# Second round's last counts and chain steps one slot earlier, second expert's token pieces turned at the first expert's last product

## What is computed

```python
def _moe_ref(x, w_gate, w1, w2):            # N, D = 1536, 512; E, F = 8, 1024
    cap = N // E                            # 192 tokens for each expert
    logits = x @ w_gate
    order = np.argsort(-logits.flatten())
    ...                                     # best (token, expert) pair first; full experts are passed over
    for e in range(E):
        mask = assigned == e
        h = np.maximum(x[mask] @ w1[e], 0.0)
        out[mask] = h @ w2[e]

def _moe2_ref(x, w_in, w_out, alpha):       # d_ff = 2048
    h = x @ w_in
    g = np.maximum(h, 0.0) + alpha * np.minimum(h, 0.0)
    return g @ w_out
```

## Time and profile before

| | us |
|---|---|
| median of 3 runs | 648.62 (648.44 to 649.32) |
| the profiled execution | 646.13 |
| its span, first to last instruction | 644.4 |

### The profile page before, as it was taken

How to read it: one execution, slowest core, us unless ns; L and a number is a source line. 1 busy time by engine, 2 the same in 40 slices (tenths; PEclk the granted TensorE clock), 3 DMA queues, 4 the chain that set the end, 5 groups by cost and what they waited for, 6 DMA issues and landing times.

```text
span 644.4 us, 12853 instructions
## 1 busy us (share of the span) xinstructions
PE 620.3 (96%) x4926; PEld 554.2 (86%) x4933; DVE 418.6 (65%) x1148; ACT 299.7 (47%) x704; POOL 195.7 (30%) x212
## 2 busy tenths in 40 slices
PE   7899999989999999999999999999999999999994
PEld 4788897558899888899999888999988989999994
DVE  8688887988576979844759798438577520045551
ACT  5877784111122655532246554322566542346652
POOL 5988870010110342121113431201234420123322
PEclk9999999999999999999999999999999999999998
DMA  7477765525350143027103510470017610000001
GB/s 257 148 262 267 257 197 165 180 91 198 110 226 2 66 149 122 2 79 264 45 2 106 188 43 1 138 246 2 2 66 260 239 44 14 1 0 2 1 1 49
DMA packets 31284, 72.36 MB, mean 112 GB/s; under 512 B 2940, under 2 KB 3000, under 8 KB 31224
## 3 DMA queue, kind: packets, MB, share of 16 engines
q1 hardware_dynamic: 27232, 60.69, 27.3%
q0 software_dynamic: 2048, 6.29, 3.3%
q10 hardware_dynamic: 1944, 4.56, 2.0%
HBM read 65.22 MB, written 6.32 MB: 111 GB/s over the span
## 4 chain that ended last, share of the span: by engine, by line
PE 81%; DVE 5%; ACT 1%; issue 0%; POOL 0%; POOLq 0%; ACTq 0%; DVEq 0%
PE bank L1511 21%; PE bank L1500 20%; PE bank L1418 13%; PE bank L1409 13%; PE bank L1334 3%; DVE beats L906 3%; PE bank L1253 2%; PE bank L1217 1%; PE bank L1199 1%; PE bank L1387 1%; PE bank L1365 1%; PE bank L1274 1%; DVE ties L915 1%; PE bank L1349 0%; POOL out L603 0%
## 5 line engine op out<-in xcount | busy, mean ns | idle before, releaser
L580 POOL TENSOR_TENSOR wi_lo<-w_in,wi_hi 128x512 fp32r<-128x512 f32 x64 | 85.7, 1342 | 278.8 <-ACT wi_hi L706 278.8
L906 DVE TENSOR_SCALAR beats<-rank_row,key 128x512 bf16<-128x512 f32 (+11 forms) x173 | 105.7, 636 | 13.0 <-PE bank L1336 13.0
L1511 PE MATMUL bank<-wo_hi,g_lo 128*128 128x512 f32 x192 | 76.0, 396 | 0.0
L1511 PE MATMUL bank<-wo_lo,g_hi 128*128 128x512 f32 x192 | 75.8, 395 | 0.0
L1511 PE MATMUL bank<-wo_hi,g_hi 128*128 128x512 f32 x192 | 75.5, 393 | 0.0
L1156 DVE SCALAR_TENSOR_TENSOR g<-bank,g_neg 128x384 f32<-128x384 f32 x64 | 35.5, 555 | 57.4 <-ACT g_neg L760 57.1
L758 ACT ACTIVATE g_neg<-bank 128x384 f32<-128x384 f32 x64 | 31.4, 491 | 79.8 <-PE bank L1500 79.8
L1500 PE MATMUL bank<-y_hi,wi_hi 128*128 128x384 f32 x256 | 58.2, 349 | 1.3 <-DVE g L1156 1.3
L642 ACT ACTIVATE prob<-neg_s,neg_max 128x260 f32<-128x260 f32 x96 | 48.9, 510 | 18.7 <-DVE neg_max L817 17.3
L732 ACT ACTIVATE h_t<-bank 128x192 f32<-128x192 f32 x64 | 21.1, 330 | 74.1 <-PE bank L1409 74.1
L1500 PE MATMUL bank<-y_hi,wi_lo 128*128 128x384 f32 x256 | 55.3, 337 | 0.0
(11 more groups left out here) (163 smaller groups left out, 1340.7 us busy)
## 6 DMA issues: line engine op xcount, KB each, us to landing
w_a<-moe_w SPq DMA_DIRECT2D x8, 1024.0 KB, 5.1
w_a<-moe_w SPq DMA_DIRECT2D x4, 2048.0 KB, 10.2
w_b<-moe_w SPq DMA_DIRECT2D x8, 1024.0 KB, 5.1
w_b<-moe_w SPq DMA_DIRECT2D x4, 2048.0 KB, 10.3
k_raw<-k_t SPq DMA_DIRECT2D x11, 512.0 KB, 5.1
q_raw<-q_t SPq DMA_DIRECT2D x11, 512.0 KB, 3.7
w_in<-moe_w_in SPq DMA_DIRECT2D x8, 512.0 KB, 5.3
w_out<-moe_w_out SPq DMA_DIRECT2D x8, 512.0 KB, 5.6
```

Source lines behind the costliest of these rows:

```text
L580: nc.gpsimd.tensor_tensor(out=wi_lo[:, f % 2, :, :], in0=w_in[:, :, f * P:(f + 1) * P], in1=wi_hi[:, f % 2, :, :].bitcast(F32), op=ALU.sub ...
L906: return nc.vector.tensor_scalar(out=beats[:, c % 3, lo:hi], in0=rank_row[:, lo:hi], scalar1=key[:, c:c + 1], scalar2=None, op0=op)
L1511: last = nc.tensor.matmul(DOWN_BANK[t][:, :], a[:, f % 3, t * P:(t + 1) * P], w[:, f % 2, :], start=(f == 0 and n == 0), stop=(f == FC - 1 ...
```

## The change

On PE, in expert 0: the counts of blocks 8 to 11 move to the places behind products 4 (8 and 9) and 5 (10 and 11) instead of products 4, 5 (9 and 10) and 6 (11); in the numbers of the code, done = 5 and 6 instead of 5, 6 and 7. `across(1)` moves from done = 8 to 7, `before_and_loads(1)` from 8.5 to 8, `pick_tokens(1)` from 10 to 9.5. The turning of expert 1's tokens is cut in two: piece 0 goes into the middle of product 11 (done = 11.5), piece 1 stands right behind it, and the four matmuls on zeros are gone. On ACT the copy of piece 0 stands behind `store_keys(2)`, before the last `y_hi` copy, and that of piece 1 behind `load_row(2)`. On DVE the second part of `picks(1)` no longer has `y_rest(0, 0)` in front of it.

```diff
@@ scalar engine
-            def copy_x(r):
+            def copy_x(r, pieces=range(TURNS)):
...
-                for k, (t, rows) in enumerate(ROWS[e]):
+                for k in pieces:
+                    t, rows = ROWS[e][k]
                     act.wait_ge(x_turned, TURNS * r + k + 1)
...
-                if r < 2:
+                if r == 0:
                     copy_x(r)
...
                     if r == 0 and m == 2:
                         store_keys(2)
+                        copy_x(1, (0,))
                 if r == 0:
                     load_row(2)
+                    copy_x(1, (1,))
@@ vector engine, experts(0)
                     fill_expert(1)
-                    picks(1, PARTS[0])
+                    for tiles in PARTS:
+                        picks(1, tiles)
                     y_rest(0, 0)
-                    picks(1, PARTS[1])
                     token_numbers(1)
@@ tensor engine
+            def turn_piece(r, k):
+
+                j, e = r // 2, r % 2
+                t, rows = ROWS[e][k]
+                pe.wait_ge(gathered[e][k], 16 * (j + 1))
...
+                for c in range(DC):
+                    last = nc.tensor.transpose(x_bank(r, k)[:, c * width:(c + 1) * width], x_g[rows, t, c * P:(c + 1) * P],
+                                               ident[rows, rows])
+                last.then_inc(x_turned, 1)
+
             def turn_tokens(r):
...
+                for k in range(TURNS):
+                    turn_piece(r, k)
...
-            SECOND_ROUND = {1: (3,), 2: (4,), 3: (5, 6), 4: (7,), 5: (8,), 6: (9, 10), 7: (11,)}
+            SECOND_ROUND = {1: (3,), 2: (4,), 3: (5, 6), 4: (7,), 5: (8, 9), 6: (10, 11)}
...
+                    if done == 7:
+                        across(1)
                     if done == 8:
-                        across(1)
-                    if done == 8.5:
                         before_and_loads(1)
-                    if done == 10:
+                    if done == 9.5:
                         pick_tokens(1)
                     if done == 11:
                         turn_keys(2)
+                    if done == 11.5:
+                        turn_piece(1, 0)
...
                 if j == 0:
-                    keep_clock(4, DOWN_BANK[2])
-                    turn_tokens(1)
+                    turn_piece(1, 1)
```

More of the change, by code:

```diff
@@ L1370, in _ @@
             pe.wait_ge(consts_ready, CONSTS)
-            def turn_tokens(r):
[L1374 to L1389, removed]
+            def turn_piece(r, k):
+                j, e = r // 2, r % 2
+                t, rows = ROWS[e][k]
+                pe.wait_ge(gathered[e][k], 16 * (j + 1))
+                if r == 0:
+                    pe.wait_ge(row_copied, 3 + k + 1)
+                elif e:
+                    wait_above(pe, o_copied, GT * j)
+                else:
+                    pe.wait_ge(y_copied, DC * r - 1 + k)
+                    if k == 0 and j < NG - 1:
+                        pe.wait_ge(keys_copied, KEYS_BESIDE_FFN[j - 1] - 1)
+                width = rows.stop - rows.start
+                for c in range(DC):
+                    last = nc.tensor.transpose(x_bank(r, k)[:, c * width:(c + 1) * width], x_g[rows, t, c * P:(c + 1) * P],
+                                               ident[rows, rows])
+                last.then_inc(x_turned, 1)
+            def turn_tokens(r):
+                for k in range(TURNS):
+                    turn_piece(r, k)
             def product(r, k):
```

## The result

The changed kernel takes 649.22 us (median of 20 runs, 647.05 to 651.91) against 647.74 us for the kernel before, measured beside it (20 runs, 646.15 to 649.32). The ratio is 1.0026 with a 95% interval of 1.0015 to 1.0036: slower by 1.7 us (1.0 to 2.3), where 0.75 us less was forecast.

The account below looks back on a forecast made before the run. PE, busy 96% of the span, was taken to bound the kernel. The filler's 0.81 us less 0.05 for the tie gave 0.75, so 648.62 becomes 647.9 us; range 646.9 to 649.1, the forecast's own 647.6 to 648.1.

Parts of the forecast that it names:

- the quarter of a microsecond forecast at count 11 and at `across`: Moved routing steps in expert 0: inputs ready 0.25 us ahead at both places, so PE does not wait.
- they take nothing off PE: Routing steps one slot earlier in expert 0: same sum on PE up to product 11, only slack of 1.30 us.
- the gathers in time: Middle of product 11: piece 0 landed 1.4 us before PE asks, 0.0 with the slowest landing.
- the filler's 0.8 us: Seam from expert 0 to 1: gain 0.8 us, exactly the matmuls on zeros; expert 1 starts at 176.5 against 177.28.
- What is late next: Third round's first count: keys' load issued 0.4 us later, a tie with PE at 182.3, costing 0 to 0.1 us.
- It shares them after the change too: Keys' load beside expert 1's weights: DMA engines shared as before, earlier weights leave the keys' share alone.
- the 6.2 us: Keys' load for the third round: issue to landing taken over unchanged from the kernel before.
- the gain is eaten at count 0: Rival, third round's first count: keys' load alone 0.8 us late, 648.6 us, no change; chance 13%.
- a load issued later than 175.3: Sign of being wrong: `load_row` going out after 175.3, where the keys' load was forecast near 175.2.
- Keys stored late and holding ACT: Rival, ACT before expert 1: late store delays `load_row(2)` and piece 1's copy; 649.8 us or more; chance 8%.
- The clock at the seam: Rival, start of expert 1: without zeros products 0 to 3 run at 1.2 GHz, 5.4 us more, 653.3; chance 2%.
- More than the filler gained: Rival, gathers at the seam: landing later without the profiler, so gain 1.2 to 1.7 us, 646.9; chance 17%.

Follow-up runs that it names:

- turning only: The changed kernel with the second round's routing steps put back to their old places; ratio 1.0030 to the kernel before.
- zeros gone: The kernel before with only the four matmuls on zeros behind product 11 of expert 0 taken out; ratio 0.9991.
- keys first: The changed kernel with w2 of expert 1 issued behind the keys' load and `load_row(2)` ahead of the last `y_hi` copy; ratio 0.9975 to the kernel before.
- both pieces: keys first with piece 1 also turned in the middle of product 11, its copy ahead of the last `y_hi` copy; 645.7 us, ratio 0.9965 to the kernel before.
- minimal: The kernel before with zeros gone, `load_row(2)` ahead of the last `y_hi` copy and w2 behind that copy, without moved steps, pieces or cut copies; ratio 0.9993.
- the first four experiments: The kernel before without zeros, or with only the steps moved; the changed kernel with steps put back, or with w2 held back; ratios 0.9991, 1.0015, 1.0030, 1.0006.
- w2 behind keys: The changed kernel with one wait on SP, so w2 of expert 1 is issued behind the last `y_hi` copy; 647.89 us, ratio 1.0006 to the kernel before.
- before with w2 behind: The kernel before with only w2 of expert 1 issued behind the last `y_hi` copy of expert 0; ratio 1.0001.
- before again: The kernel before, unchanged, run once more for a second trace; no ratio given, first count 10.49 us behind the issue of the keys' store.

## Why the prediction was wrong

**What held.** That PE bounds the stretch; that all of the moved steps find their inputs (the quarter of a microsecond forecast at count 11 and at `across` sufficed); that they take nothing off PE; the gathers in time; the seam cheaper by the filler's 0.8 us (0.89 in the trace); no fall of the clock at the seam; that the keys' load is what comes late next, with no room left.

**The step that failed** is in "What is late next": "It shares them after the change too", and with it the 6.2 us taken over for a load that was issued in another order. The load took 7.5 and 7.7 us and PE waited 1.9 and 2.1 us where I had 0 to 0.1. The first trace's 1.89 us are 1.26 for the later landing (7.46 against 6.2), 0.44 for a term that I had mis-sized (from DVE's start on the landed keys to the count are 1.34 us, 183.94 to 185.28, where I put 0.9, although I took 1.4 us a block a few sentences later), and some 0.2 for a load issued 0.5 to 0.6 us later instead of 0.4 and the tie. Even with the old 6.2 us the count would have been at 10.4 behind the store and the gain about 0.1. The sum was 0.8 gained at the seam and 1.9 lost at the count, 1.1 us slower (11.63 against 10.49 behind the keys' store; 11.84 in the second trace), which lies in the interval of the runs, 1.0 to 2.3. I had seen that both transfers share the engines, and that the weights move up by 1.3 us. I had not looked at which of them was issued first: before, the keys went out 0.2 us ahead of w2; after, 1.7 behind. I named this cost as a rival ("the gain is eaten at count 0") and priced it as a load 0.8 late. DVE started 1.5 us later than forecast (10.29 us behind the store, where 2.6 and 6.2 make 8.8), and the longer first block came on top. One of my own signs of being wrong, a load issued later than 175.3, was met by a hair (175.32), but that was the small part.

The Trainium skill's page "DMA: Bandwidth & Descriptors", section "Queues, rings and completion order", on which I leaned, says that each engine takes turns between queues packet by packet. The rows disagree with how I read it: 1.20 MB of weights moved in 3 us, 104% of the engines' time, with the keys' load already issued. Once both move they agree with it: in the kernel before, 178 to 180 us, 100 packets of the keys passed beside 99 of the weights. The keys' share is three times as large since their packets hold 6 KB against 2 KB (0.61 MB against 0.20). The same section says that SP and ACT have no descriptor generator of their own. A common one that works in order of issue would explain that w2 ahead of the keys delays them. It would not by itself explain that their first bytes come 3.8 us behind their issue with w2 0.4 us ahead (turning only), 1.7 ahead (the change) and 0.1 behind (zeros gone). No run here tests it. That w2's place costs the time is shown; how it does so stays open.

**The other rivals.** Keys stored late and holding ACT: not seen; the load went out at once behind product 11 in both traces. The clock at the seam: in thirteen traces no window of 5 us between 155 and 235 us is below 1.00, with seams that hold 0.7 us of idle time and waits of up to 2.1 us. More than the filler gained: not in the changed kernel, whose two traces show 0.8 us at the seam and no more.

**What stays open.** The runs move more than the traces in some kernels: 1.6 us against 0.8 for keys first, 2.3 against 1.4 for both pieces, 1.7 against 1.1 for the change; in minimal they move less, 0.5 against 0.9. The granted clock of single runs lies between 0.986 and 0.998, and in the traces the low stretches, apart from the kernel's end, are at 15 to 30 or 145 to 155 us, ahead of all that is edited. The mean over the runs was 0.9918 for the changed kernel and 0.9940, 0.9927 and 0.9932 for the kernel before on three chips. Within one kernel a run whose mean clock is lower by 0.001 is some 0.3 us longer. An estimate with that slope, all runs taken to one clock, leaves the change 0.9 us slower (0.4 to 1.3, against the 33 runs of before that came with the first experiments), keys first 1.3 faster, minimal 0.8 faster and both pieces 1.9 faster. So about half of the 1.7 us may go with the clock and not with the wait. On the chip of the first four experiments the kernels with pieces turned in product 11 had the lower clock (0.9921 and 0.9922, against 0.9938 to 0.9940 for the others); on the chip of keys first that did not come back (0.9938 and 0.9925 with the pieces, 0.9927 before). I take that for scatter, but no experiment settled it.

## What to carry to other kernels

When an edit lets a transfer go out earlier, list what is issued within the next few microseconds on every queue, and see whose place it takes: a large load that nobody waits for soon can be put ahead of a smaller one on which the next step hangs. The cure is one wait that holds the unhurried transfer back, and the urgent one issued as early as its data allow. Slack given to one side is worth nothing until something uses it: the moved steps cost 1 us alone and seem to pay only where both pieces go into the product.

## What the runs showed of the hardware

- Two transfers on different queues didn't share the engines from their issue on. With w1's second half (1 MB) issued 0.6 to 2.1 us ahead and w2 held back, the keys' first bytes came 4.2 to 4.3 us behind the issue of that half (2.2 us behind their own issue in w2 behind keys, 3.4 in keys first). With the half 0.2 to 0.4 us ahead and w2 just behind the keys they came 2.6 to 3.8 us behind their own issue, with the half and 2 MB of w2 ahead 3.8 to 4.2, and with nothing large ahead 1.0 (minimal).
- With the keys 0.34, 0.18, 0.14 and 0.10 us ahead of w2 they landed after 6.4, 6.2, 6.8 and 7.1 us (before with w2 behind, before, before again, zeros gone), one trace each. An order of issue decided by so little gave no steady landing.
- Once both queues had work moving, they passed packet for packet, 100 of the keys beside 99 of the weights in 2 us, and the one with 6 KB packets got three times the bytes of the one with 2 KB (before, 178 to 180 us).
- Cutting an accumulation of f32 products with eight transposes cost PE nothing that the trace shows: product 11 with both pieces takes 3.58 us from start to the next product (174.35 to 177.93), of which 0.89 us are the transposes (175.74 to 176.63). The 2.69 us left are what an uncut product 11 takes in zeros gone (2.70, 173.61 to 176.31).
